# Where the combine weights are turned and how the first projection group runs, in a fused attention and mixture-of-experts kernel

## The reference, cut to what matters

```python
# soft mixture: phi 512x32, w1 8x512x1024, w2 8x1024x512
logits = x @ phi
d = softmax(logits, axis=0)                 # over tokens, per slot
slot_input = (d.T @ x).reshape(E, 4, 512)
slot_out[e] = relu(slot_input[e] @ w1[e]) @ w2[e]
c = softmax(logits, axis=1)                 # combine weights, 2304x32
x2 = c @ slot_out.reshape(32, 512)
# projection: w_in 512x2048, w_out 2048x512
h = x2 @ w_in
g = h * clip(h + 3, 0, 6) / 6
out = g @ w_out
```

## Time and profile before

| | us |
|---|---|
| median of 3 runs (lowest, highest) | 435.21 (434.94, 436.25) |
| the profiled execution | 436.03 |
| its span, first to last instruction | 434.3 |

### The profile page before, as it was taken

How to read it: one execution, slowest core, us unless ns; L and a number is a source line. 1 busy time by engine, 2 the same in 40 slices (tenths; PEclk the granted TensorE clock), 3 DMA queues, 4 the chain that set the end, 5 groups by cost and what they waited for, 6 DMA issues and landing times.

```text
span 434.3 us, 9701 instructions
## 1 busy us (share of the span) xinstructions
PE 422.4 (97%) x3507; PEld 342.5 (79%) x3507; DVE 232.5 (54%) x700; ACT 212.1 (49%) x600; POOL 69.9 (16%) x112
## 2 busy tenths in 40 slices
PE   7899999999999999999999999999999999999996
PEld 7688788888888886635777888888888888888885
DVE  3557696677669666323454544444534435444442
ACT  3778776878677731001755344343444343343431
POOL 1233133222213310200865000000000000000000
PEclk9999999999999999999999999999999999999999
DMA  9958998899798489999900101010100101010101
GB/s 176 221 161 263 238 249 221 231 261 226 206 240 248 134 282 326 381 388 398 357 5 1 48 2 48 0 48 0 48 0 4 44 0 48 0 48 0 49 2 48
DMA packets 75492, 61.37 MB, mean 141 GB/s; under 512 B 57792, under 2 KB 57792, under 8 KB 75456
## 3 DMA queue, kind: packets, MB, share of 16 engines
q1 hardware_dynamic: 73376, 60.37, 46.1%
q10 hardware_dynamic: 2080, 0.52, 0.7%
HBM read 56.16 MB, written 4.72 MB: 140 GB/s over the span
## 4 chain that ended last, share of the span: by engine, by line
PE 88%; DVE 5%; ACT 4%; issue 2%; DMA 1%; POOL 0%; DVEq 0%
PE probs_turned L1046 23%; PE out_turned L1046 22%; PE scores L809 7%; PE probs_turned L818 4%; PE out_turned L834 4%; PE scores L1028 4%; PE scores L983 3%; PE routes L865 3%; PE scores L963 3%; PE out_turned L838 3%; PE turns L849 2%; PE turns L792 2%; ACT probs L420 2%; PE turns L782 2%; PE scores L775 2%
## 5 line engine op out<-in xcount | busy, mean ns | idle before, releaser
L727 DVE SCALAR_TENSOR_TENSOR g<-u,scores 128x512 f32<-128x512 f32 x72 | 49.6, 689 | 106.7 <-ACT u L463 106.7
L468 ACT ACTIVATE g_hi<-g 128x512 fp32r<-128x512 f32 x72 | 45.5, 632 | 114.6 <-PE out_turned L1046 113.8
L420 ACT ACTIVATE probs<-probs,rowmin 128x128 f32<-128x128 f32 (+1 forms) x160 | 62.0, 391 | 6.4 <-DVE rowmin L536 6.3
L1046 PE MATMUL probs_turned<-w_out_hi,g_hi 128*128 128x512 f32 x144 | 57.3, 398 | 1.5 <-ACT g_hi L468 1.2
L1046 PE MATMUL probs_turned<-w_out_lo,g_hi 128*128 128x512 f32 x144 | 56.9, 395 | 0.0
L1046 PE MATMUL probs_turned<-w_out_hi,g_lo 128*128 128x512 f32 x144 | 56.1, 390 | 0.0
L1046 PE MATMUL out_turned<-w_out_hi,g_lo 128*128 128x512 f32 x144 | 56.1, 390 | 0.0
L1046 PE MATMUL out_turned<-w_out_hi,g_hi 128*128 128x512 f32 x144 | 56.1, 390 | 0.0
L1046 PE MATMUL out_turned<-w_out_lo,g_hi 128*128 128x512 f32 x144 | 56.1, 389 | 0.0
L733 DVE TENSOR_TENSOR g_lo<-g,g_hi 128x512 fp32r<-128x512 f32 x72 | 50.7, 705 | 2.8 <-ACT g_hi L468 2.8
L463 ACT ACTIVATE u<-scores 128x512 f32<-128x512 f32 x72 | 41.9, 581 | 2.1 <-PE scores L1028 2.1
(11 more groups left out here) (141 smaller groups left out, 652.8 us busy)
## 6 DMA issues: line engine op xcount, KB each, us to landing
weight_ring<-in_moe_w_dram SPq DMA_DIRECT2D x30, 1024.0 KB, 7.2
out_dram<-y SPq DMA_DIRECT2D x18, 256.0 KB, 2.0
q_in<-in_q_dram SPq DMA_DIRECT2D x16, 256.0 KB, 4.2
v_in<-in_v_dram SPq DMA_DIRECT2D x16, 256.0 KB, 3.9
weight_ring<-in_moe_w_in_dram SPq DMA_DIRECT2D x8, 512.0 KB, 12.3
weight_ring<-in_moe_w_out_dram SPq DMA_DIRECT2D x4, 1024.0 KB, 15.7
k_in<-in_k_dram SPq DMA_DIRECT2D x14, 256.0 KB, 4.5
weight_extra<-in_moe_w_dram SPq DMA_DIRECT2D x2, 1024.0 KB, 8.3
```

The source lines that it names most:

```text
L420: act.activation(probs[0:R, m % 2, h, :], probs[0:R, m % 2, h, :], ACT.Exp, bias=rowmin[0:R, m % 2, h:h + 1], scale=-1.0, accum_out=rsum[0 ...
L468: act.activation(g_hi[:, p % 2, :], g_sb[:, p % 4, :], ACT.Copy).then_inc(ghi_ready, 1)
L727: dve.scalar_tensor_tensor(out=g_sb[:, p % 4, :], in0=u_sb[:, p % 2, :], scalar=6.0, in1=bank[p % 4], op0=ALU.min, op1=ALU.mult).then_inc( ...
L1046: ins = pe.matmul(bank[4 + kk][:, :], g[:, p % 2, cols], w[:, c, :], start=(p == 0 and i == 0 and a == 0), stop=(p == FPAIRS - 1 and i == ...
```

## The change

`COMBINE_AT` goes: w2's eight pieces run through. The 20 token tiles are now turned in five fills of four tiles, one PSUM bank each (`fill_bank`), and ACT copies them, not DVE. Fills 0 and 1 stand right behind w2 in the place of `occupy(3)`, fill 2 in the place of `occupy(2)`, fill 3 behind `compact(0)` in the place of `occupy(4)`, fill 4 behind `hidden(1)`; the `occupy(8)` ahead of chunk 0 becomes `occupy(3)`. DVE splits batches 2 and 3 in w2's time into a second `combine4` buffer.

Group 0 runs by halves of 256 columns: `spread_wp(0)` signals each half, DVE copies two halves, and relu, gate, high and low are each two instructions of 256 columns. The second half of its h lies in another bank. In chunk 0 `project` becomes `project_rows` for one kk at a time, with the matmuls that need `w_out_lo` last; `hidden(2)` and `(3)` stand between group 0's two rows, `compact(1)` ahead of group 1, `spread_wp(2)` and `(3)` between group 1's rows, `hidden(4)` and `(5)` between group 2's rows. w_out is loaded in eight halves of quarters, and w_in's second half comes ahead of w_out's second quarter.

```diff
-            load_w_out(1)
             load_w_in(1)
+            load_w_out(1)
...
+                for i in range(2):
+                    first = n * WROWS + i * WROWS // 2
+                    sp.dma_start(wout_sb[n][:, i * WROWS // 2:(i + 1) * WROWS // 2, :], ...)\
+                      .then_inc(wout_in[2 * n + i], 16)
...
-                for b in range(BATCHES):
-                    if n == max(COMBINE_AT, COMBINE_AT - 1 + b):
-                        turn_combine(b)
-            occupy(3, bank[0])
+            turn_combine(0)
+            turn_combine(1)
...
-            occupy(2, bank[0])
+            turn_combine(2)
             pe.wait_ge(so_ready, 1)
-            pe.wait_ge(comb_copied, BATCHES)
...
+            def turn_combine(f):
+                pe.wait_ge(comb_ready, (4 * f + 3) // TILES + 1)
+                for n in range(4 * f, 4 * f + 4):
+                    (b, tt), R, at = divmod(n, TILES), rows_of(n), token(n) - token(4 * f)
+                    ins = pe.transpose(fill_bank(f)[:, at:at + R], comb4[b // 2][0:R, b % 2, tt]..., ident[0:R, 0:R])
+                ins.then_inc(comb_turned, 1)
...
+            def copy_combine(f):            # ACT
+                act.wait_ge(comb_turned, f + 1)
+                at, width = token(4 * f), token(4 * f + 4) - token(4 * f)
+                act.activation(comb_t[:, at:at + width], fill_bank(f)[:, 0:width], ACT.Copy).then_inc(comb_copied, 1)
...
+            def first_group():              # ACT; DVE has its counterpart
+                act.wait_ge(first_h, 1)
+                act.activation(u_sb[:, 0, 0:CHUNK], hidden_bank(0, 0, 0), ACT.Relu, bias=3.0).then_inc(first_relued, 1)
+                act.wait_ge(h_done, 1)
+                act.activation(u_sb[:, 0, CHUNK:2 * CHUNK], hidden_bank(0, 0, 1), ACT.Relu, bias=3.0).then_inc(relued, 1)
+                act.wait_ge(first_gated, 1)
+                act.activation(g_hi[:, 0, 0:CHUNK], g_sb[:, 0, 0:CHUNK], ACT.Copy).then_inc(first_high, 1)
+                act.wait_ge(gated, 1)
+                act.activation(g_hi[:, 0, CHUNK:2 * CHUNK], g_sb[:, 0, CHUNK:2 * CHUNK], ACT.Copy).then_inc(ghi_ready, 1)
...
+            copy_combine(0)                 # ACT's order behind w2
+            copy_combine(1)
+            copy_combine(2)
             split_high(0)
+            first_group()
+            relu(1, 1)
+            copy_wp(1)
             split_high(1)
-            copy_wp(1)
-            relu(0, 0)
-            chunk(0, False)
+            copy_combine(3)
+            for n in range(1, FPAIRS):
+                if n == 3:
+                    copy_wp(3)
+                high(n, n)
+                relu(n + 1, (n + 1) % FPAIRS)
+                if n == 1:
+                    copy_combine(4)
+                for p in {1: (2,), 2: (3, 4)}.get(n, (n + 2,)):
+                    if p < FPAIRS:
+                        split_high(p)
...
             compact(0)
-            occupy(4, bank[0])
+            pe.wait_ge(comb_copied, 3)
+            turn_combine(3)
...
-            for p in range(PARTS):
-                hidden(p, 0, p)
-            occupy(8, bank[5])
-            chunk(0, False)
+            hidden(0, 0, 0)
+            hidden(1, 0, 1)
+            turn_combine(4)
+            occupy(3, bank[4])
+            for p in range(FPAIRS):
+                if p == 1:
+                    pe.wait_ge(comb_copied, 4)
+                    compact(1)
+                if p >= 4:
+                    hidden(p + 2, (p + 2) // FPAIRS, (p + 2) % FPAIRS)
+                project_rows(p, 0, p, 0)
+                if p == 0:
+                    hidden(2, 0, 2)
+                    hidden(3, 0, 3)
+                if p == 1:
+                    pe.wait_ge(comb_copied, FILLS)
+                    spread_wp(2)
+                    spread_wp(3)
+                if p == 2:
+                    hidden(4, 0, 4)
+                    hidden(5, 0, 5)
+                project_rows(p, 0, p, 1)
```

More of the change, by code:

```diff
@@ L104, in layer_program @@
     pick = place("pick", [P, QUADS, 6, SLOTS], tail + 17536, f32r)
[L105 to L106 removed]
+    comb4 = [place(f"combine4_{i}", [P, 2, TILES, 2, 2, SLOTS], tail + (21760, 9216)[i]) for i in range(2)]
+    so = place("slot_out", [P, D], tail + 14336)
     hid = place("hid", [P, CHUNK], tail + 27392)
@@ L745, in chunk @@
                     n = FPAIRS * m + p
[L746 to L753, removed]
                     if not (last and p == FPAIRS - 1):
                         gate(n + 1, (p + 1) % FPAIRS)
-                    if not ahead:
-                        low(n, p)
-                    if p == 0 and not (isinstance(m, int) and m == 0):
+                    low(n, p)
+                    if p == 0:
                         out_rows(m - 1)
             split_compact(0)
-            copy_wp(0)
-            gate(0, 0)
-            chunk(0, False)
+            copy_wp_first(0)
+            copy_wp_first(1)
+            first_group()
+            gate(1, 1)
+            for n in range(1, FPAIRS):
+                if n == 2:
+                    split_compact(1)
+                if n == 3:
+                    copy_wp(2)
+                if n in (1, 3):
+                    low(n, n)
+                gate(n + 1, (n + 1) % FPAIRS)
+                if n not in (1, 3):
+                    low(n, n)
             with dve.Fori(1, CHUNKS - 1) as m:
@@ L1034, in project, with product @@
                 first = isinstance(m, int) and m == 0
-                pe.wait_ge(ghi_ready, n + 1)
-                pe.wait_ge(glo_ready, n + 1)
+                if not first and p == 0:
+                    pe.wait_ge(y_copied[kk], m)
+                def product(i, g, w, a):
+                    c = 2 * p + i
+                    return pe.matmul(bank[4 + kk][:, :], g[:, p % 2, i * CHUNK + kk * P:i * CHUNK + (kk + 1) * P],
+                                     w[:, c, :], start=(p == 0 and i == 0 and a == 0),
+                                     stop=(p == FPAIRS - 1 and i == 1 and a == 2))
@@ L1037, in project @@
                 if first:
[L1038 to L1041 removed]
                     for i in range(2):
[L1043 to L1052 removed]
+                        if n == 0 and i == 0:
+                            pe.wait_ge(first_low, 1)
+                        else:
+                            pe.wait_ge(glo_ready, n + 1)
@@ new lines, in project_rows @@
+                        product(i, g_hi, w_hi, 0)
+                        product(i, g_lo, w_hi, 1)
+                    for i in range(2):
+                        pe.wait_ge(lo_split, 2 * p + i + 1)
+                        ins = product(i, g_hi, w_lo, 2)
+                else:
+                    pe.wait_ge(ghi_ready, n + 1)
+                    pe.wait_ge(glo_ready, n + 1)
+                    for i in range(2):
+                        for a, (g, w) in enumerate(((g_hi, w_hi), (g_hi, w_lo), (g_lo, w_hi))):
+                            ins = product(i, g, w, a)
@@ L1056, in chunk @@
                     n = FPAIRS * m + p
[L1058 to L1069 removed]
+                    if p + 2 < FPAIRS:
                         hidden(n + 2, m, p + 2)
```

129 lines of the change are left out of this document (58 added, 71 removed).

## The result

| | before | after |
|---|---|---|
| median of 4 runs, us (lowest, highest) | 435.07 (434.71, 436.25) | 430.43 (429.92, 430.84) |
| ratio, 95% interval | | 0.9886 [0.9873, 0.9898] |
| the profiled execution, us | 436.03 | 429.92 |
| its span, us | 434.3 | 428.2 |

The changed kernel is 1.1% faster, and 430.5 had been forecast. The spans differ by 6.1 us, more than the medians, so the first thing to look at is where the change can have acted at all. PE starts w2 at 183.92 us, where it did at 185.25, although nothing ahead of it was changed: 1.33 us of the 6.1 belong to the execution and not to the change. In the 13 profiles of this study, all with the same work ahead of w2, that start lies anywhere between 183.45 and 185.25. From here on every event is therefore counted from the start of w2 in its own profile, which takes this spread out.

A forecast was written before the change was run, and what follows sets the result against it. PE, busy 97% of the span, was taken as the bound. Group 4's first projection was to come 4.17 - 0.48 + 1.20 = 4.89 us earlier, less 0.2 for unknown costs: 435.2 - 4.7 = 430.5 us, range 429.9 to 433.0.

The forecast's parts named there:

- w2 in one piece: w2 without combine's transposes takes 14.14 us, ends 3.36 us earlier; its last half lands 1.4 us before use.
- The transposes in the waits: Behind w2: fills overfill the waits by 0.31 plus 0.1 us for short tiles; compact(0) starts at 202.0.
- wp and group 0: hidden(0) at 206.2; half-width stations bring the projection 2.23 us later, not 3.35; it starts 4.17 us earlier.
- From group 0 to group 4: First projection to group 4's: 15.46 us of PE work, 0.48 added by hidden(2) and (3); the 1.20 us stall goes.
- a chain that ends in a tie: Before group 4: the chain from hidden(4) ends at 223.9, just when PE could start, with no margin.
- a sign of being wrong: Any group between 1 and 4 starting behind a PE idle of over 0.3 us would show the prediction wrong.
- unknown costs of another kind: Joins of split groups, the tie at group 4 and fillers hiding less than thought: 0.2 us taken off 4.89.
- The loads: Swapped load order: w_in's second half ends at 210.1, letting compact(1), which wants it from 211.9, stand ahead of group 1.
- The feared wait of ACT: Slower case: ACT waits at split_high(2) for w_out's third eighth; slower if it lands over 6.7 us late; chance 0.05.
- The clock: Rival: transposes behind w2 drop PE to the lower pace for 9.3 us; time 435.1, no change; chance 0.05.
- The loads did not bind: Rival judged: loads bind behind PE until the first projection, compact(0) waits; about 434.5 us; chance 0.04.
- The new wait: Rival: halves bring nothing, ACT's queue keeps the 1.20 us stall at group 4 or earlier; 432.6 us; chance 0.18.

The follow-up runs named there:

- e1: Changed kernel with combine's fills 0 to 3 turned between w2's pieces again and fillers back in the waits behind w2; 433.07 us.
- e6: Changed kernel with low ahead of the next gate for groups 4 and 5, and fills placed so that no wait is overfilled; 430.47 us.
- e9: Changed kernel with low ahead of the next gate on DVE for groups 4, 5 and 6 too; 430.00 us.
- e2: Changed kernel with group 0's relu, gate, high and low in full width of 512 columns, its h in one bank; 431.31 us.
- e3: Changed kernel with hidden(4) and hidden(5) in front of group 3, not between group 2's rows; 431.45 us.
- e7: Changed kernel with POOL writing zeros to w_out_lo from row chunk 4 on where it subtracted, for measurement only; 430.06 us.
- e5: Changed kernel with low ahead of the next gate on DVE for groups 4 and 5 too; 430.48 us.
- e4: Changed kernel with the loads as before: w_out in whole quarters, its second quarter ahead of w_in's second half; 430.77 us.
- e11: Changed kernel with fitted fills and low ahead of the next gate for groups 4 to 6, but group 0 in full width; 430.83 us.
- e8: Changed kernel with 16 further transposes behind fills 0 and 1, 24 in a row in all; 432.21 us in one run.

## Why the prediction was right

**w2 in one piece.** Forecast 14.14 us, measured 13.94; e1 shows the mechanism. The last half of w2 landed at 180.9 + 15.0 = 195.9 in the changed kernel, 1.1 us ahead of its use, against 1.4 forecast.

**The transposes in the waits.** Forecast: overfilled by 0.41 in all, and `compact(0)` 16.75 us behind w2's start (202.0 - 185.25). Measured 16.74 (200.66 - 183.92), which is closer than its terms: w2 was 0.20 shorter than forecast, and the waits behind it took 2.80 us where they had taken 2.21 (202.76 to 204.97), so they were overfilled by 0.59. The fills with a short tile took 0.68 and 0.71, not 0.59. e6 agrees on the price of the overfilling: fitted fills gave 0.48.

**wp and group 0.** `hidden(0)` was forecast 20.95 behind w2's start and came at 20.67, since PE got through spreading sooner than I had counted. From there to the projection 2.23 was forecast and 2.20 measured. So the projection started 4.48 us earlier, not 4.17: 0.31 to the good.

**From group 0 to group 4.** This is the step that was mis-sized. I had the 1.20 us stall go entirely, with a chain that ends in a tie; 15.46 us from the first projection to group 4's. It took 15.90. The profile shows PE idle for 0.41 of it, over the 0.3 that the prediction named as a sign of being wrong. The wait cost more than that: with no idle the stretch takes 15.30 (e9), so PE's own work had been forecast 0.16 too long and the wait cost 0.60. The term behind it is `low`: I took 1.01 us from the earlier trace rows as its price beside POOL, and it was 1.66, 1.82, 1.55 and 1.45 in groups 1 to 4. At 1.01, `low(4)` would have ended at 222.19 and left PE almost nothing to wait for. The row that I used was one sample of a duration that goes from 0.7 to 1.85 with the phase of POOL's subtractions (e2, e3, e7); the kernel before has 1.22 at group 2. And the order on DVE placed it behind a gate that had to wait (e5, e9).

That order was in the old stall too, and the prediction missed it. It took ACT for the releaser, as the bracket in the earlier trace rows says. But the `g_hi` that ended last there, at 228.60, was group 5's; group 4's was ready at 226.55. What group 4 needed and got last was `low(4)`, which stood behind `gate(5)`:

```profile
227.07 0.69 DVE L727 SCALAR_TENSOR_TENSOR g<-u,scores 128x512 f32<-128x512 f32 x1 [1.35 <-ACT u L463]
```

It began at 227.68 and ended at 228.69, 0.09 ahead of PE.

The two errors nearly cancel: 4.89 + 0.31 - 0.44 = 4.76. The forecast of 4.7 us had taken 0.2 off for unknown costs of another kind, so its closeness is partly luck; its terms are right to 0.3 and 0.4 us.

**The loads.** I wrote that the new order is what lets `compact(1)` stand where it does. e4 does not bear it out: with the order and the halving undone, `compact(1)` did not wait and group 4 came 0.07 later. But its projection was 0.60 late, about the room that the chunk had (212.2 to 212.8); the old order with halved loads would be close to a tie, and was not run. I had compared the landing of w_in's last chunk with the start of `compact(1)` and not with the use of that chunk, 1.4 us later. The feared wait of ACT for w_out's third eighth did not come, but narrowly: it landed at 196.6 + 13.6 = 210.2 and was wanted at 210.36.

**How the 4.76 us divide.** Undone singly, the parts cost 2.79 (combine out of w2), 0.53 (halves), 0.73 (the place of `hidden(4)` and `(5)`) and 0.07 (loads) at group 4, together 4.12. The 0.64 that are left are not shown to belong to any one part. Candidates are the rows taken one at a time, with `w_out_lo` last, which was not tried by itself, and what the single parts mask of each other, as e2 and e11 show for the halves.

**The rivals.** The clock did not fall (e8). The loads did not bind (e1, e4). The new wait was there, but smaller than in that rival: it took 0.60 us and not 2.3, the halves did bring their gain, and it was DVE's order and POOL, not ACT's queue, that kept it.

## What to carry to other kernels

Work that nobody waits for belongs into an engine's real waits, and it is worth its full time there only while it fits the wait: 1.27 us of transposes in a wait of 0.87 lost 0.4 again. Follow a gain to the next point where two chains meet before counting it. Half of one part's gain was eaten at group 4, and a first repair only moved the wait to group 6. Where a duration on such a chain varies with what another engine happens to do, bound it from the longest row and not from a typical one.

## What the runs showed of the hardware

**DVE waits for POOL where both read SBUF.** A DVE subtraction of two SBUF operands, 128x512, takes 0.68 to 0.69 us alone and beside a POOL instruction that only writes, and up to 1.85 us beside POOL subtractions of SBUF operands that follow each other every 1.41 us (e6, e7). Single subtractions, two of the changed kernel and one of e2 (duration in ns, start), show where the time goes:

```profile
L405 POOL TENSOR_TENSOR w_out_lo<-weight_ring,w_out_hi x1: 1297/1297/1297, 220.8 to 220.8; 128x512 fp32r<-128x512 f32 x1
L405 POOL TENSOR_TENSOR w_out_lo<-weight_ring,w_out_hi x1: 1743/1743/1743, 222.0 to 222.0; 128x512 fp32r<-128x512 f32 x1
...
L403 POOL TENSOR_TENSOR w_out_lo<-weight_ring,w_out_hi x1: 1300/1300/1300, 222.1 to 222.1; 128x512 fp32r<-128x512 f32 x1
```

In the changed kernel `low(4)` starts at 221.18, in the middle of the first, and ends at 222.63, 0.5 us behind that one's end at 222.1. In e2 it starts at 223.05 and ends at 223.95, again 0.5 behind the end at 223.4. In e6 it starts with a subtraction, at 220.51, and takes the full 1.85. So `low` takes the rest of the subtraction under way and about 0.55 us more. The subtraction behind it then takes 1.74 to 1.77 us in these three in the place of 1.30: POOL waits in its turn.

The Trainium skill, SBUF — State Buffer, section "Who interferes with whom", says that such a DVE instruction contends with a GpSimd instruction that reads SBUF and not with one that only writes, and calls what the two engines share an exclusive lock. The trace agrees: the surplus of `low` runs from nothing to about 1.2 us, less than one of POOL's subtractions, 1.28 us at the shortest.

**Transposes keep PE's pace.** After 24 in a row (3.02 us), the matmuls behind them ran at full pace, with the clock granted in full, the level of 2.4 GHz (e8). The statement of the Trainium skill, TensorE: Matmul & The Clock Gate, section on the PE-mode transpose, that was weighed in the prediction is not borne out by any run here, with other matmuls before and behind the stretch. Sixteen in a row took 0.109 us each, four 0.147, and four with one of 64 rows among them 0.68 to 0.83 together.

**The start of w2 varies by 1.8 us** from one execution to another with the same code ahead of it. Single spans are too coarse for parts worth half a microsecond; distances between events of one profile are not.
